# Seven score items computed early and parked in device memory, with GpSimd making both halves of twenty weight pieces

## The reference, cut to what matters

```python
scores = scale * np.matmul(q, k.transpose(0, 1, 3, 2))       # 4 batches, 8 heads, 576 x 576
kth = np.partition(scores, -32, axis=-1)[..., -32:-31]       # keep the 32 largest of each row
attn = np.exp(np.where(scores >= kth, scores, -1e9) - scores.max(-1, keepdims=True))
x = (attn / attn.sum(-1, keepdims=True)) @ v                 # then to (2304, 512)
h = x @ w_in;  g = np.maximum(0.01 * h, h);  x = g @ w_out            # 512 -> 2048 -> 512
h = x @ w_in2; g = piecewise((h + 1)**2 / 4 between -1 and 1, h above) # and once more
out = g @ w_out2
```

## Time and profile before

| what | value |
|---|---|
| median of 3 runs | 1164.52 us (1164.34 to 1165.52) |
| the profiled execution | 1163.93 us, span 1162.1 us |
| PE busy | 1092.6 us (94%) |
| DVE busy | 877.2 us (75%) |
| ACT busy | 791.6 us (68%) |
| POOL busy | 464.8 us (40%) |
| DMA moved | 295.52 MB |
| a piece's store (512 KB), issue to landing | median 5.0 us |

### The profile page before, as it was taken

The page is one execution under the profiler, slowest core; times in us unless marked ns, Lnnn a source line. Parts: engine busy times, 40 slices in busy tenths (PEclk is TensorE's granted clock), DMA queues, the critical chain, the costliest instruction groups (busy, mean ns, idle before and its releaser), DMA issues.

```text
span 1162.1 us, 21227 instructions
## 1 busy us (share of the span) xinstructions
PE 1092.6 (94%) x7568; PEld 1002.3 (86%) x7568; DVE 877.2 (75%) x1921; ACT 791.6 (68%) x1827; POOL 464.8 (40%) x493
## 2 busy tenths in 40 slices
PE   5457998899999999999999999999999999999998
PEld 3336887799988998899999879989998999999998
DVE  7999999889889998999979989888993005300234
ACT  7887999787788877887869868778885224322332
POOL 5654468552264432643225434225532234222322
PEclk9679999999999999999999999999999999999999
DMA  7988988697657788788667667565555677787764
GB/s 247 351 337 298 366 307 311 217 377 252 234 201 237 246 307 289 274 291 293 237 232 245 220 218 247 203 211 192 169 195 210 213 257 253 254 285 251 256 246 139
DMA packets 90680, 295.52 MB, mean 254 GB/s; under 512 B 10064, under 2 KB 13776, under 8 KB 90576
## 3 DMA queue, kind: packets, MB, share of 16 engines
q1 hardware_dynamic: 86544, 289.45, 71.2%
q10 hardware_dynamic: 4032, 4.72, 1.1%
HBM read 255.85 MB, written 38.27 MB: 253 GB/s over the span
## 4 chain that ended last, share of the span: by engine, by line
PE 69%; DVE 18%; ACT 5%; issue 3%; POOL 3%; DMA 1%; SPq 0%; POOLq 0%; ACTq 0%; DVEq 0%
PE ps_f L928 19%; PE ps_f L936 18%; PE ps_f L929 18%; DVE top L1211 8%; DVE work L1215 7%; PE ps_av L887 6%; PE ps_s L848 3%; PE ps_t L864 2%; DVE part_r L1238 2%; PE ps_t L870 2%; DMA raw<-wd 1%; PE ps_t L848 1%; POOL gate L741 1%; ACT probs L1056 1%; ACT probs L1048 1%
## 5 line engine op out<-in xcount | busy, mean ns | idle before, releaser
L1211 DVE MAX8 top<-work 128x8 f32<-128x576 f32 x432 | 310.2, 743 | 0.2
L928 PE MATMUL ps_f<-xy,w_ring 128*128 128x384 f32 (+2 forms) x896 | 289.3, 323 | 5.7 <-ACT gate L1115 2.0
L928 PE MATMUL ps_f<-gate,w_ring 128*128 128x384 f32 (+2 forms) x896 | 285.2, 318 | 0.0
L936 PE MATMUL ps_f<-gate,w_ring 128*128 128x384 f32 (+2 forms) x896 | 280.9, 314 | 4.1 <-POOL gate L741 4.0
L936 PE MATMUL ps_f<-xy,w_ring 128*128 128x384 f32 (+2 forms) x896 | 281.1, 314 | 1.6 <-POOL xy L751 1.1
L929 PE MATMUL ps_f<-xy,w_ring 128*128 128x384 f32 (+2 forms) x896 | 280.3, 313 | 0.0
L929 PE MATMUL ps_f<-gate,w_ring 128*128 128x384 f32 (+2 forms) x896 | 279.8, 312 | 0.0
L1215 DVE MATCH_REPLACE8 work<-top,work 128x576 f32<-128x576 f32 x288 | 213.3, 740 | 0.0
L741 POOL TENSOR_TENSOR gate<-part_r,gate 128x384 fp32r<-128x384 f32 (+2 forms) x112 | 101.3, 905 | 244.0 <-ACT gate L1115 243.9
L928 PEld LDWEIGHTS ps_f<-xy,w_ring 128*128 128x128 f32 x896 | 169.7, 189 | 19.9 <-issue 10.1
L928 PEld LDWEIGHTS ps_f<-gate,w_ring 128*128 128x128 f32 x896 | 169.2, 189 | 6.5 <-issue 6.2
(11 more groups left out here) (85 smaller groups left out, 1842.0 us busy)
## 6 DMA issues: line engine op xcount, KB each, us to landing
w_ring<-w_split SPq DMA_DIRECT2D x408, 512.0 KB, 4.2
w_split<-w_ring SPq DMA_DIRECT2D x40, 512.0 KB, 6.3
raw<-wd SPq DMA_DIRECT2D x64, 256.0 KB, 5.8
w_split<-xy SPq DMA_DIRECT2D x24, 512.0 KB, 5.0
v_sb<-vd SPq DMA_DIRECT2D x32, 320.0 KB, 5.7
kq<-kqd SPq DMA_DIRECT2D x16, 480.0 KB, 4.9
kq<-kqd SPq DMA_DIRECT2D x15, 416.0 KB, 3.6
out_t<-y_acc ACTq DMA_DIRECT2D x12, 192.0 KB, 4.3
```

Of the source, the lines that this page charges most:

```text
L928: pe.matmul(out, w[:, 0, m], high, start=first, stop=False)
L936: mm = pe.matmul(out, w[:, 0, m], low, start=False, stop=end)
L1211: op = dve.max(top[:, t % TOP_SLOTS, 8 * r:8 * r + 8], source(t, r))
```

## The change

Items 13 to 19 are scored in steps 18, 8, 9, 11, 12, 13 and 16 instead. Their slots of `scores` are still taken then, so ScalarE copies their scores into one of three stages, which lie in tiles that have no use before the dense layers (`part_r`, `part_o`, `y_acc`); SP stores each stage to a new device tensor `s_spilled` in the next step, and loads it into its slot of `scores` in step 19, 21, 23, 25, 26, 28 or 30 (`REFILL_AT`). VectorE waits for that load (`spill_loaded`) instead of for ScalarE's copy. The order of the q and k groups follows the new order of scoring. In a step a parked item is scored last on TensorE, and copied behind `exponential` on ScalarE. The first 20 of the 24 `PREP` pieces get their high half from GpSimd too (`by_pool_alone`).

```diff
+SPILLED_AT = {13: 18, 14: 8, 15: 9, 16: 11, 17: 12, 18: 13, 19: 16}
+STAGES = 3
 def score_step(it):
+    if it.n in SPILLED_AT:
+        return SPILLED_AT[it.n]
...
+REFILL_AT = {ITEMS[n - S_SLOTS].last + EXP_LAG + 1: n for n in SPILLED}
...
+def by_pool_alone(i):
+    return i < len(PREP) - PREP_HELD
...
+            def store_spilled(it):
+                a = SPILL_ORDER.index(it.n)
+                sp.wait_ge(scores_copied, 2 * PLACE[it.n] + 2)
+                sp.dma_start(spilled(it, s_dram[a, :, :, :]),
+                             spilled(it, stages[a % STAGES])).then_inc(spill_stored[a % STAGES], 16)
+
+            def load_spilled(it):
+                a = SPILL_ORDER.index(it.n)
+                sp.wait_ge(spill_stored[a % STAGES], 16 * (a // STAGES + 1))
+                sp.wait_ge(kept, ITEMS[it.n - S_SLOTS].last + 1)
+                sp.dma_start(spilled(it, scores[:, it.n % S_SLOTS, :, :]),
+                             spilled(it, s_dram[a, :, :, :])).then_inc(spill_loaded[it.n % S_SLOTS], 16)
...
             for s in range(len(PLAN)):
-                if s in KQ_LOAD_AT:
-                    load_kq(KQ_LOAD_AT[s])
+                for gp in KQ_LOAD_AT[s]:
+                    load_kq(gp)
+                if s:
+                    for it in SPILL_OF[s - 1]:
+                        store_spilled(it)
+                if s in REFILL_AT:
+                    load_spilled(ITEMS[REFILL_AT[s]])
...
             def low_piece(i):
                 j, s = JOB_OF[PREP[i]], i % SPLIT_SLOTS
-                pool.wait_ge(high_split, j + 1)
+                if by_pool_alone(i):
+                    pool.wait_ge(raw_loaded[j % RAW_SLOTS], 16 * (j // RAW_SLOTS + 1))
+                    if i >= SPLIT_SLOTS:
+                        pool.wait_ge(split_stored[s], 16 * (i // SPLIT_SLOTS))
+                    pool.tensor_copy(split[:, s, 0, :], raw[:, j % RAW_SLOTS, :]).then_inc(high_by_pool, 1)
+                    pool.wait_ge(high_by_pool, i + 1)
+                else:
+                    pool.wait_ge(high_split, high_by_act(j))
                 pool.tensor_tensor(split[:, s, 1, :], raw[:, j % RAW_SLOTS, :], split[:, s, 0, :].bitcast(F32),
                                    ALU.subtract).then_inc(low_split, 1)
...
                     if s in OUT_AT:
                         transpose(OUT_AT[s])
+                    for it in SPILL_OF[s]:
+                        score(it)
...
             def copy_scores(it):
+                k = PLACE[it.n]
                 dst = scores[:, it.n % S_SLOTS, :, :]
-                if it.n == 0:
+                if it.n in SPILLED_AT:
+                    a = SPILL_ORDER.index(it.n)
+                    dst = stages[a % STAGES]
+                    need(act, spill_stored[a % STAGES], 16 * (a // STAGES))
...
                     if t is not None:
                         exponential(t)
+                    for it in SPILL_OF[s]:
+                        copy_scores(it)
                     for a in direct_pieces(s):
                         high_direct(a)
                     for i in prep_pieces(s):
-                        high_piece(i)
+                        if not by_pool_alone(i):
+                            high_piece(i)
```

More of the change, by code:

```diff
@@ L420, in prep_pieces, with high_by_act @@
     return range(max(0, s), max(0, min(held, s + 2)))
+def by_pool_alone(i):
+    return i < len(PREP) - PREP_HELD
+def high_by_act(j):
+    return j + 1 - sum(by_pool_alone(i) for i in range(len(PREP)) if JOB_OF[PREP[i]] <= j)
 def lowered_pieces(s):
@@ L533, in build @@
         later = xy[:, 1, :, :, :].rearrange("p h c n -> p (h c n)")
+        stages = [part_r[:, :, :].rearrange("p a n -> p (a n)"), part_o[:, :, :].rearrange("p a n -> p (a n)"),
+                  y_acc[:, :, :].rearrange("p a n -> p (a n)")]
+        stages = [a[:, 0:2 * S].rearrange("p (h n) -> p h n", h=2) for a in stages]
         split = later[:, 0:SPLIT_SLOTS * 2 * PIECE].rearrange("p (a h n) -> p a h n", a=SPLIT_SLOTS, h=2)
@@ L552, in build @@
         out_stored = sem("out_stored")
+        spill_stored = [sem("spill_stored%d" % a) for a in range(STAGES)]
+        spill_loaded = [sem("spill_loaded%d" % a) for a in range(S_SLOTS)]
         zeroed = sem("zeroed")
@@ L587, in score_halves, with spilled @@
         def score_halves(it):
-            return [ps_s, ps_f[:, 0:2, :] if it.n < SCORED_EARLY else ps_late]
+            return [ps_s, ps_f[:, 0:2, :] if PLACE[it.n] < SCORED_EARLY else ps_late]
+        def spilled(it, where):
+            return where[:, 0:it.tiles, :]
         def x_parts(gp):
@@ L626, in load_kq @@
             def load_kq(gp):
[L627 to L631, removed]
-                first, end = kq_span(gp)
-                sp.dma_start(kq[:, gp % KQ_SLOTS, first:end], kqd[gp, :, first:end]).then_inc(kq_loaded[gp % KQ_SLOTS], 16)
+                if KQ_PLACE[gp] >= KQ_SLOTS:
+                    old = KQ_ORDER[KQ_PLACE[gp] - KQ_SLOTS]
+                    if old >= FIRST_ROUNDED:
+                        sp.wait_ge(kq_low_done, 2 * (old - FIRST_ROUNDED + 1))
+                    else:
+                        sp.wait_ge(scores_done, 2 * LAST_PLACE[old] + 2)
+                first, end = kq_span(gp)
+                sp.dma_start(kq[:, kq_slot(gp), first:end], kqd[gp, :, first:end]).then_inc(kq_loaded[kq_slot(gp)], 16)
+            def store_spilled(it):
[9 more added lines that the diff above has]
+                             spilled(it, s_dram[a, :, :, :])).then_inc(spill_loaded[it.n % S_SLOTS], 16)
             def load_v(gp):
@@ L757, in low_kq @@
                 slot = kq_split[:, gp % KQ_HALVES, :, first:end]
-                pool.tensor_tensor(slot[:, 1, :], kq[:, gp % KQ_SLOTS, first:end], slot[:, 0, :].bitcast(F32),
+                pool.tensor_tensor(slot[:, 1, :], kq[:, kq_slot(gp), first:end], slot[:, 0, :].bitcast(F32),
                                    ALU.subtract).then_inc(kq_low_done, 1)
@@ L1107, in read_bank @@
                     act.wait_ge(gate_low_done[old.layer], old.in_layer + 1)
+                if u.h == 0:
+                    for a in range(min(STAGES, len(SPILLED))):
+                        act.wait_ge(spill_stored[a], 16 * len(range(a, len(SPILLED), STAGES)))
                 slot = u.h % G_SLOTS
@@ L1283, in _ @@
                         dve.wait_ge(scores_copied, t + 1)
+                    elif t == it.first and it.n in SPILLED_AT:
+                        earlier = [n for n in SPILLED if n <= it.n and n % S_SLOTS == it.n % S_SLOTS]
+                        dve.wait_ge(spill_loaded[it.n % S_SLOTS], 16 * len(earlier))
                     elif t == it.first:
-                        dve.wait_ge(scores_copied, 2 * it.n + 2)
+                        dve.wait_ge(scores_copied, 2 * PLACE[it.n] + 2)
                     top8(t, 0)
```

57 lines of the change are left out of this document (36 added, 21 removed).

## The result

The changed kernel takes 1170.76 us (median of 5 runs, 1169.53 to 1172.67), the kernel before in the same comparison 1165.43 us (5 runs, 1164.34 to 1165.63): ratio 1.0050, 95% interval 1.0035 to 1.0065. It is 5.3 us, 0.5%, slower. The forecast was 1166.6 us, with "slower" its likeliest sign (0.43). The time lies inside the range of 1160.5 to 1171.5, but just above the main case's own range of 1163.5 to 1170, so the sizes of the steps need explaining.

The account below looks back on a forecast made before the run. VectorE, full up to its add of unit 23 at 161 us, was taken to hold TensorE's unit 24. A 5.6 us delay less 3.5 saved gave +2.1 on 1163.93, and 0.6 to the median: 1166.6 us, range 1160.5 to 1171.5.

Parts of the forecast that it names:

- main case: ScalarE's waits for parked scores outweigh later savings: 1166.6 us, own range 1163.5 to 1170, chance 0.50.
- rival (b): GpSimd and the DMAs become the bound of steps 6 to 16: 1171 us, chance 0.16.
- rival (d): TensorE's lead ahead of unit 24 does count, 8.7 us: 1156 us, chance 0.02.
- TensorE idle for some 6 us just ahead of it: Sign of being right: TensorE stands idle some 6 us just ahead of VectorE's add of unit 23, at about 166.5.
- Steps 17 and 19: Copies of item 19 (steps 16, 17) and item 13 (18, 19) make VectorE later: +2.2 and +1.8 us.
- Step 13: Steps 12 and 13: copies of items 17 and 18 delay VectorE by +0.9 us (0.5 to 1.5).
- step 9: Steps 8 and 9: item 14's copies come 1.0 us late, less 0.5 slack: +0.5 us.
- Steps 14 and 15: No parked item, two pieces less on ScalarE, VectorE's old 1.17 us wait to be won: -0.4 us (-1.2 to 0).
- What costs nothing: The parked items' DMAs, 3.5 MB each way, fit in free queue time or are hidden by TensorE's lead over unit 24.
- What the change saves behind unit 23: Behind 161 us VectorE's three `part_o` waits go, the 2.92 us wait stays: -3.5 us (-1.2 to -7).
- (a): Parked scores keep TensorE's clock at 2.4 GHz, so the waits shrink: 1161 us, chance 0.18.
- (c): No visible effect, stalls and savings both small (delay 2.5, saving 2.5): 1164.5 us, chance 0.12.

Follow-up runs that it names:

- e1: Changed kernel with nothing parked, GpSimd making both halves of twenty pieces: 1162.38 us, 0.9982 of the kernel before.
- e4: Changed kernel with parked items stored and loaded with 8 of 576 columns: 1169.77 us, 1.0050 of the kernel before.
- e5: Kernel before, scores of items 13 to 16 cut to 8 of 288 columns on TensorE and ScalarE: 1165.69 us, ratio 1.0009.
- e6: Kernel before, scores of items 17 to 19 cut to 8 of 288 columns on TensorE and ScalarE: 1162.85 us, ratio 0.9982.
- e8: Changed kernel parking only items 17 to 19, in steps 8, 10, 12, copied a step later and stored one more later: 1160.58 us, 0.9962 of before.
- e10: Changed kernel with the parked score ahead of the values product in steps 9 and 13: 1169.77 us, 1.0036 of the kernel before.
- e11: Changed kernel, parked scores cut to 8 of 288 columns, their DMAs to 8 of 576: 1164.83 us, 0.9998 of the kernel before.

## Why the prediction was right, and where its sizes were off

**The range.** It held partly by luck. The main case's own range ended at 1170 us, short of the 1170.76 measured. The upper end of 1171.5 us was there for rival (b), GpSimd and the DMAs as the bound, which e1 and e4 refute.

**What bounds the kernel.** The conclusion was right, the place was read too late. e5 shows that time won ahead of unit 24 is not kept, and rival (d), TensorE's whole lead, is out. In all thirteen profiles the end follows the add of unit 23 by 997 to 1002 us. But the sign "TensorE idle for some 6 us just ahead of it" did not come: TensorE has three waits, 2.0 us in sum (0.91 at 165.35, 0.30 at 167.26, 0.75 at 170.16). Before there was no wait to point at, since it went from transposes into unit 24 at 161.34 without a gap. Of the lead, 1.9 us are waited away already in step 24, where ScalarE waits for VectorE (3.03 us before, 3.47 now) and TensorE for ScalarE to empty a bank; before, and in the changed kernel:

```profile
113.17 0.39 PE L928 MATMUL ps_f<-xy,w_ring 128*128 128x256 f32 x1 [1.97 <-ACT gate L1115]
121.14 0.39 PE L993 MATMUL ps_f<-xy,w_ring 128*128 128x256 f32 x1 [3.86 <-ACT gate L1190]
```

**What the change delays.** The mechanism was right, the sum too small: 8.2 us measured for 5.6.
- Steps 17 and 19: 2.34 and 1.99 us for 2.2 and 1.8. Right.
- Step 13: 1.24 us for 0.9; step 9: 0.2 for 0.5 (its close at 43.53 for 42.94, of which 0.43 were there before). Together as expected.
- Steps 14 and 15: this is the term that failed. It was put at -0.4 ("no parked item, two pieces less"); the wait grew from 1.17 to 2.83 us, +1.7, which makes 2.1 of the 2.6 us that the sum is short. (With the 1.69 and 1.89 us that e5 and e6 show for the old wait, the growth is 0.9 to 1.7.) For a parked item in an odd step, TensorE's values product stands ahead of its score, and I counted item 15's such wait as nothing and item 18's not at all. It was 3.18 us.
- GpSimd: 0.6 us taken, with 0.75 us for the copy. The copy is 0.61 us, next to ScalarE's 0.62, and e1 shows no late multiplication that reaches VectorE. In the changed kernel one is 1.4 us late, in step 12 (55.79 for a close at 53.36), but TensorE's own scores run to 56.86 and hide it all but 0.1 us. The Trainium skill (GPSIMD Engine Reference, Elementwise) gives 769 ns for its tight loop; the measured copy is shorter, and the measurement decides. Its section Engine selection, by which one-input operations on GpSimd run at roughly line rate, agrees with the row. Taken apart, GpSimd's halves are a gain of 2.1 us of span: 0.8 at the add, where the wait of 1.17 us goes, and 1.3 behind it, where the clock of the last section makes 1.6.

**What costs nothing.** Right: e4. SP did wait for item 13's store in step 19 (issue of the load at 100.26, the store's at 95.59), and e4 without the length of these transfers is no faster. The items parked are four of 590 KB and three of 295 KB, not five and two: 3.2 MB each way, as the 302.01 - 295.52 = 6.5 MB show.

**What the change saves behind unit 23.** This term failed too: 3.5 us forecast, 1.8 measured, and nearly all of it by another wait than I named. The three for `part_o` went from 1.25, 0.98 and 1.30 to 1.17, 0.62 and 1.30 us, 0.4 together. The fourth, of 2.92 us, which I left in place, became 1.27. That 1.65 us goes with TensorE's clock at this place, as the last section shows, and no run ties it to the change. In e6 the waits for `part_o` sum to 2.8 us with their smaller neighbours, so they are little tied to the scores of items 17 to 19. Against the medians (1170.76 less 1165.43, or less the 1164.2 to 1164.9 of the later comparisons, so 5.3 to 6.5 us) the delay of 8.2 us leaves 1.7 to 2.9 us that came back; of these the profile names only the 0.4 and the clock's.

**The rivals.** (a) The clock: 0.84 granted from 25 to 100 us instead of 0.75, so it did rise, but item 19's scores in step 16 still ran at 1.2 GHz: 0.84 us for the first matmul and 0.68 for the last, where the earlier trace rows have 0.85 and 0.68 at 1.2 GHz. That was the point named, and it decided against (a). The Trainium skill (TensorE: Matmul & The Clock Gate, What's actually happening) has the default throttled and activity lifting it; the trace agrees in the direction, but the place that mattered did not get it. (b) GpSimd and DMA as the bound: the time came close to its 1171 us by another way; e1 and e4 exclude both. (c) asked for a delay of 2.5 us; it was 8.2.

**What stays open.** Whether more score banks, or a shorter parked score, would make all seven items pay, and what that prize is: e5 shows none ahead of unit 24, and e6 priced half of the work behind it at some 2 us. Whether e8's parked items themselves win anything over e1: 1.8 us by the medians, 0.2 at the add and 0.9 behind it in the two profiles, and the two intervals just touch (0.9974 and 0.9973).

## What to carry to other kernels

Work moved into an engine's idle time still needs somebody to pick up the result, and the one who does it waits in order: cost the round trip at the reader, with what stands ahead of it on the producer, and not the work at the engine that had room. A result buffer that holds one item turns "copy it later" into the same wait at the other end, so put such work only where the buffer is idle until the late copy. And before valuing saved work, look for the next point at which that engine must wait for a full one; cutting the work short, as in e5 and e6, prices it with one run, once the trace has said how much of the work the cut took.

## What the runs showed of the hardware

TensorE's granted clock differs between profiles at a place where the program is the same. Behind the same idle time of 1.76 us and the same scores, the sixteen matmuls of a values product took 3.71 us in the kernel before and 2.37 us with GpSimd's halves alone; first the timeline of before, then that of e1:

```profile
199.89 0.37 PE L848 MATMUL ps_s<-kq_split 64*128 64x288 f32 x1 [1.76 <-ACT p_rem L1076]
201.16 3.71 PE L887 MATMUL ps_av<-p_t,v_sb 128*64 128x320 f32 x16
```

```profile
199.09 0.37 PE L913 MATMUL ps_s<-kq_split 64*128 64x288 f32 x1 [1.76 <-ACT p_rem L1148]
200.08 2.37 PE L952 MATMUL ps_av<-p_t,v_sb 128*64 128x320 f32 x16
```

From 195 to 205 us the clock is 0.83 in the one and 1.00 in the other, and VectorE's wait behind it 2.92 and 1.28 us. e10 has such a dip (2.91 us of wait at 215.81) and so has e5 (2.96 at 211.34), the others not (1.25 to 1.28). This is 1.6 us of a difference of spans. Whether it belongs to the execution or to the kernel isn't shown, since each kernel has one profile: the dip is in two of the three kernels that park nothing and leave the halves to ScalarE, and in one of the ten others. Over the runs of the kernel before the mean clock goes from 0.977 to 0.987. A difference of 2 us between two profiles should be traced to its place before it is given a cause.

A matmul's time falls less than its columns: the eight of an item took 1.24 us at 2.4 GHz with 288 columns and 0.62 us with 8 (e5, e6), and 2.29 and 1.03 us at 1.2 GHz (e11).
